# Windowed attention on one core: transposes two groups behind the scores, value products three groups behind

## The reference

```
scores = scale * np.matmul(q, k.transpose(0, 1, 3, 2))
keep = is_sink | in_window            # pos < n_sink, or 0 <= query - key < window
scores = np.where(keep, scores, -1000000000.0)
a = np.exp(scores - np.max(scores, axis=-1, keepdims=True))
a = a / (np.sum(a, axis=-1, keepdims=True) + 1e-09)
return np.matmul(a, v).astype(np.float32)
```

## Time and profile before

| | us |
|---|---|
| median of 3 runs | 871.35 (870.74 to 871.47) |
| the profiled execution, its own time | 870.85 |
| its span in the profile | 869.0 |
| TensorE busy in the span | 846.8 (97%) |
| VectorE busy | 615.8 (71%) |
| ScalarE busy | 400.8 (46%) |
| GpSimd busy | 170.0 (20%) |

### The profile page before, as it was taken

The page is one execution under the profiler, slowest core; times in us unless marked ns, Lnnn a source line. Parts: engine busy times, 40 slices in busy tenths (PEclk is TensorE's granted clock), DMA queues, the critical chain, the costliest instruction groups (busy, mean ns, idle before and its releaser), DMA issues.

```text
span 869.0 us, 13947 instructions
## 1 busy us (share of the span) xinstructions
PE 846.8 (97%) x4512; PEld 728.7 (84%) x4512; DVE 615.8 (71%) x1221; ACT 400.8 (46%) x739; POOL 170.0 (20%) x255
## 2 busy tenths in 40 slices
PE   5988999999999999999999999999999999999998
PEld 4666788888888888888999989998899989998896
DVE  6888779989898999885655656566565565655655
ACT  4888675445864457873144134224314314422410
POOL 4666410000110012231122022022012202202100
PEclk9999999999999999999999999999999999999999
DMA  7444550000780001861353154055135224313303
GB/s 252 142 141 131 141 143 4 2 1 16 169 196 7 0 0 38 173 128 30 86 117 57 58 115 88 27 115 115 23 91 115 48 66 115 74 41 66 67 1 148
DMA packets 25191, 72.72 MB, mean 84 GB/s; under 512 B 4288, under 2 KB 5952, under 8 KB 25152
## 3 DMA queue, kind: packets, MB, share of 16 engines
q0 software_dynamic: 10720, 33.82, 21.5%
q1 hardware_dynamic: 14288, 38.04, 13.0%
q10 hardware_dynamic: 144, 0.39, 0.2%
HBM read 35.28 MB, written 3.15 MB: 44 GB/s over the span
## 4 chain that ended last, share of the span: by engine, by line
PE 94%; ACT 2%; DVE 2%; issue 1%; DMA 1%; DVEq 0%; ACTq 0%
PE banks L877 30%; PE banks L803 27%; PE banks L774 15%; PE banks L598 15%; PE banks L613 2%; ACT pool L972 2%; PE banks L679 2%; PE banks L652 2%; PE banks L685 1%; DMA prm<-params 1%; DVE x_lo L1409 0%; DVE row_den L1399 0%; DVE pool L1389 0%; PE banks L655 0%; DVE mask L1300 0%
## 5 line engine op out<-in xcount | busy, mean ns | idle before, releaser
L1649 DVE SCALAR_TENSOR_TENSOR pool<-banks,p_norm,pool 128x512 f32<-128x512 f32 x180 | 133.5, 748 | 66.7 <-PE banks L877 64.9
L877 PE MATMUL banks<-w_hi,g_lo 128*128 128x512 f32 x384 | 150.6, 392 | 0.0
L877 PE MATMUL banks<-w_lo,g_hi 128*128 128x512 f32 x384 | 150.5, 392 | 0.0
L877 PE MATMUL banks<-w_hi,g_hi 128*128 128x512 f32 x384 | 149.3, 389 | 0.0
L1190 ACT ACTIVATE g_hi<-pool 128x384 fp32r<-128x384 f32 x96 | 50.5, 526 | 190.8 <-DVE pool L1629 139.2
L803 PE MATMUL banks<-x_hi,w_lo 128*128 128x384 f32 x256 | 86.0, 336 | 0.0
L803 PE MATMUL banks<-x_hi,w_hi 128*128 128x384 f32 x256 | 85.9, 335 | 0.0
L803 PE MATMUL banks<-x_lo,w_hi 128*128 128x384 f32 x256 | 85.8, 335 | 0.0
L877 PEld LDWEIGHTS banks<-w_hi,g_lo 128*128 128x128 f32 x384 | 72.0, 188 | 15.2
L877 PEld LDWEIGHTS banks<-w_hi,g_hi 128*128 128x128 f32 x384 | 72.2, 188 | 13.6
L877 PEld LDWEIGHTS banks<-w_lo,g_hi 128*128 128x128 f32 x384 | 72.0, 188 | 13.8
(11 more groups left out here) (136 smaller groups left out, 1743.0 us busy)
## 6 DMA issues: line engine op xcount, KB each, us to landing
w_raw<-weights SPq DMA_DIRECT2D x48, 512.0 KB, 4.4
w_lo<-w_raw POOLq DMA_DIRECT2D x48, 512.0 KB, 5.4
w_lo<-w_sum POOLq DMA_DIRECT2D x15, 384.0 KB, 4.0
pool<-kT SPq DMA_DIRECT2D x8, 400.0 KB, 4.2
pool<-v SPq DMA_DIRECT2D x8, 384.0 KB, 3.0
out<-pool SPq DMA_DIRECT2D x12, 256.0 KB, 2.4
pool<-qT SPq DMA_DIRECT2D x7, 384.0 KB, 3.4
w_lo<-pool POOLq DMA_DIRECT2D x2, 384.0 KB, 4.9
```

What stands on the lines that cost most here:

```text
L877: mm = pe.matmul(banks[:, bank, :], g[:, s, f * SUP + at:f * SUP + at + P], w_cols(w, p2 * SLOT + DOWN_AT[f], DM), start=(f == 0 and n == ...
L1649: dve.scalar_tensor_tensor(out=to, in0=d_bank, scalar=share, in1=to, op0=ALU.mult, op1=ALU.add)\
```

## The change

Transposes run two groups behind the scores instead of one (TURN_LAG = 2), value products three instead of two (VALUES_LAG = 3). A third probability buffer, prob_third, is laid into weight memory that is still unused then (w_hi from slot 6 on), so the exponentials of g wait for turn(g-3). GpSimd waits once for each group instead of once for each two units. VectorE's period has another order: copy_second(g-3) first, then masks 0 and 1 of g, the x_lo part for g-4 (at the end instead where it is the first part of a batch), one invert for all four units of g-1, masks 2 and 3. At the end, values(21) and turn(22) stand ahead of start_up(0), and ScalarE's copy_first(23) ahead of reciprocal(0).

```diff
+        prob_third = sb("prob_third", [P, 4 * WIDE + P], at=w_hi_at + mybir.dt.size(f32) * 6 * WC)
+        def group_prob(g):
+            return prob_third[:, :] if g % 3 == 2 else prob_w[:, g % 3, 0:4 * WIDE + P]
...
-                        if u % 2 == 0:
-                            pl.wait_ge(den_ready, ct * (UNITS // 2) + u // 2 + 1)
+                        if u % 4 == 0:
+                            pl.wait_ge(den_ready, ct * GROUPS_A + u // 4 + 1)
...
                     scores(ct, g)
-                    if at := group_at(ct, g, 2, before):
+                    if at := group_at(ct, g, VALUES_LAG, before):
                         values(*at)
-                    if at := group_at(ct, g, 1, before):
+                    if at := group_at(ct, g, TURN_LAG, before):
                         turn(*at)
...
+                values(CT - 1, GROUPS_A - 3)
+                turn(CT - 1, GROUPS_A - 2)
                 start_up(0)
...
-                            if u % 4 == 0 and ct * GROUPS_A + g >= 2:
-                                act.wait_ge(turned, 2 * (ct * GROUPS_A + g) - 2)
+                            if u % 4 == 0 and ct * GROUPS_A + g >= 3:
+                                act.wait_ge(turned, 2 * (ct * GROUPS_A + g) - 4)
...
-                        if at := group_at(ct, g, 1, ct > 0):
+                        if at := group_at(ct, g, TURN_LAG, ct > 0):
                             copy_first(*at)
-                        if at := group_at(ct, g, 2, ct > 0):
+                        if at := group_at(ct, g, VALUES_LAG, ct > 0):
                             take_after(*at)
...
+                copy_first(CT - 1, GROUPS_A - 2)
                 split_tile_hi(0, EARLY - 1, None)
                 split_tile_neg(EARLY - 1)
                 exponential(0)
                 take_after(CT - 1, GROUPS_A - 2)
+                copy_first(CT - 1, GROUPS_A - 1)
                 reciprocal(0)
-                copy_first(CT - 1, GROUPS_A - 1)
                 take_after(CT - 1, GROUPS_A - 1)
...
-                    for u in range(4 * g, 4 * g + 4):
-                        mask_scores(ct, u)
-                    invert(ct, 4 * g, 2)
-                    if at := group_at(ct, g, 3, before):
-                        take_after(*at)
-                    invert(ct, 4 * g + 2, 2)
+                    copied = group_at(ct, g, TURN_LAG + 1, before)
+                    ended = group_at(ct, g, VALUES_LAG + 1, before)
+                    first_half = ended is not None and ended[1] % (QT // 2) == 1
+                    if copied:
+                        copy_second(*copied)
+                    mask_scores(ct, 4 * g)
+                    mask_scores(ct, 4 * g + 1)
+                    if ended and not first_half:
+                        take_after(*ended)
                     if at := group_at(ct, g, 1, before):
-                        copy_second(*at)
+                        invert(at[0], 4 * at[1], 4)
+                    mask_scores(ct, 4 * g + 2)
+                    mask_scores(ct, 4 * g + 3)
+                    if first_half:
+                        take_after(*ended)
...
+                copy_second(CT - 1, GROUPS_A - 3)
+                invert(CT - 1, 4 * (GROUPS_A - 1), 4)
+                take_after(CT - 1, GROUPS_A - 4)
+                copy_second(CT - 1, GROUPS_A - 2)
                 start_gate(0)
```

More of the change, by code:

```diff
@@ L52 @@
 ADD_AT = [7 + 4 * n for n in range(EARLY - 1)]
+TURN_LAG, VALUES_LAG = 2, 3
 LAG = 3
@@ L133, in build @@
         x_lo = sb("x_lo", [P, CT, TOK], f32r)
+        w_hi_at = free_at[0]
         w_hi = sb("w_hi", [P, STEPS, WC], f32r)
@@ L186, in build @@
         rel = prob_w[:, 1, 4 * P:6 * P]
+        prob_third = sb("prob_third", [P, 4 * WIDE + P], at=w_hi_at + mybir.dt.size(f32) * 6 * WC)
+        def group_prob(g):
+            return prob_third[:, :] if g % 3 == 2 else prob_w[:, g % 3, 0:4 * WIDE + P]
         def window_prob(u, w):
             at = WIDE * (u % 4) + (P if u % 4 >= 2 else 0)
-            return prob_w[:, u // 4 % 2, at:at + w]
+            return group_prob(u // 4)[:, at:at + w]
         prob_T = part(TURNED_AT, 4, 512)
@@ L457, in window_attention @@
                             pl.wait_ge(prob_ready, ct * UNITS + u + 1)
-                            sinks = prob_w[:, group % 2, P:P + 4 * WIDE].rearrange("p (a b) -> p a b", a=4)[:, :, 0:SINKS]
+                            sinks = group_prob(group)[:, P:P + 4 * WIDE].rearrange("p (a b) -> p a b", a=4)[:, :, 0:SINKS]
                             pl.tensor_copy(sink_prob[:, group % 2, :, :], sinks).then_inc(sinks_ready, 1)
```

## The result

The changed kernel takes 861.61 us (861.33 to 861.70, 4 runs) against 871.05 us (870.28 to 871.47, 4 runs): ratio 0.9892, 95% interval 0.9875 to 0.9909, so 9.4 us less. 11.5 were forecast; the time lies in the range, and on the side on which the gain is smaller. The profiled execution took 861.70 us, its span 859.9.

A forecast was written before the change was run, and what follows sets the result against it. TensorE, busy 97%, bounds the kernel; only its attention waits can go. Ramp 24.35 + six batches at 10.1 + end 2.5 = 87.45 us to start_up(0), against 98.93: 11.5 less, so 859.8 us, range 857 to 865.5.

The forecast's parts named there:

- TensorE's floor of 9.95 a batch: Attention's steady part: TensorE's steps without any wait sum to 9.95 us a batch, where 11.70 was measured before.
- the ping-pong on VectorE: Steady part before: VectorE stands in invert for exponentials of the same g, while ScalarE waits 14.7 us for masks.
- ScalarE's copy: copy_first out of the type 0 (narrow) period: done at 3.9, wanted at 3.96, margin nothing; charged 0.15 us a batch.
- the x_lo wait: TensorE's waits at L652 for the x_lo part, 6.5 us in seven; forecast to go, with 1.0 us margin.
- VectorE's work: Six inverts a batch become three, saving 1.0 us: busy 10.05 becomes 9.05 a batch, under TensorE's 9.95.
- The walk: Step-by-step timing of VectorE and ScalarE through one period of the new order, from its start on TensorE.
- ScalarE's copy late: Rival, chance 0.10: the type 0 margin becomes a third of a microsecond lost each period, 11.0 a batch, 865.2 us.
- The ramp: Periods 0 to 3, bound by ScalarE's and VectorE's chain: period 6 would start at 24.35 us instead of 28.70.
- The end: values(21), turn(22) and a 0.5 us wait for turn(21)'s copies between period 23 and start_up(0): together 2.5 us.
- Queues and weights at nothing: SyncE's later k load and the weight tiles, wanted 11.5 us earlier but issued 9.3 earlier, were costed at nothing.
- The port rival: Chance 0.08: every invert collides with a GpSimd multiply on the shared port, VectorE 10.5 a batch, 862.8 us.
- The x_lo wait stays, or slower: Two rivals: TensorE's x_lo wait remains, 869.5 us, chance 0.06; a two-period ring makes TensorE await copy_first, 874.9, chance 0.04.

## Why the prediction was right, point by point

- **TensorE's floor of 9.95 a batch**: right; 9.94 in the kernel with the earlier copy.
- **What holds before, the ping-pong on VectorE**: right, and shown by two kernels: with the inverse of the own group a batch stays at 11.27 to 11.30 even at the new lags. Of the 1.75 us that a batch lost before (11.70 against 9.95), the lags alone removed 0.4 (11.30), the new order with them 0.96 more (10.34), and the last 0.4 hung on the place of ScalarE's copy (9.94). The prediction named the x_lo wait and the ping-pong side by side. That the first is where the second comes out at TensorE fits the lags alone, where it was still 4.0 us, but is argued.
- **VectorE's work**: 9.05 busy us a batch were forecast, 51.76 / 6 = 8.63 came. The term that was mis-sized is the saved inverses: L1399 was charged at its median, 0.169, but its mean before was 0.250, since 15 of the 48 took over 0.2 us. "Once 0.661" is a misreading of the earlier trace rows, which gives the longest and not how many were long. "It doesn't bind" holds for its total, not for its order: 0.33 us more in front of mask 2 cost 0.38 a batch.
- **ScalarE's copy**: the place was right (a margin of nothing out of the narrow period), the size was not: charged with 0.15 us a batch, it cost 10.34 - 9.94 = 0.40, still inside the stated bounds (9.95 to 10.5 a batch). The walk has the exponentials done at about 3.4 after the narrow period's start and the copy at 3.9. In the timeline above the period starts at 25.39 and the copy, 29.21 + 0.57, ends at 4.4: mask 2 starts at 27.75, 0.35 us behind the walk. The walk gave each of the two narrow masks 0.21 us, from start to next start they take 0.40 and 0.31, so the x_lo part begins 0.32 late (why they take longer is not shown); and 0.16 us of issue lie ahead of mask 2. This is the rival "ScalarE's copy late" at somewhat over a third of its size (0.40 of 1.05 a batch).
- **The ramp**: 25.39, not 24.35. The step that failed is "as the masks now run ahead of them". The masks could not run ahead: the scores have four banks, each row of scores waits for the mask four rows back, and a row that TensorE starts out of idleness comes late. TensorE begins the first wide row at 9.31 and the mask of that row starts at 10.80; in the steady part all four rows of a group take 1.11.

```profile
10.80 0.44 DVE L1399 CUSTOM_DVE_ANT_0 pool<-banks,mask 128x272 f32<-128x272 f32 x1 [0.51 <-ACT pool L981]
...
14.62 0.52 ACT L981 ACTIVATE prob_third<-pool,row_min 128x272 f32<-128x272 f32 x1
...
15.32 0.52 ACT L981 ACTIVATE prob_third<-pool,row_min 128x272 f32<-128x272 f32 x1
15.85 0.36 ACT L992 ACTIVATE pool<-banks 128x256 f32<-128x256 f32 x1
```

  Group 2's exponentials end at 15.85 instead of 15.0, and the first copy comes late with them; period 4 starts at 18.29, where the walk has 17.25. The profile names ScalarE for the first of these waits, but its exponential was through by 9.7; that the scores were the ones awaited is read from the program's order and from when TensorE made them, not tested.
- **The end**: 2.55 against 2.5. Right. Moving start_up ahead, in the kernel with the earlier copy, won nothing.
- **Queues and weights at nothing**: right; TensorE has no idle time from 89.98 to 115.00, and the stretch from just behind the first start_up product to the end of the span is 769.9 us long (90.0 on), 770.0 before (99.0 on).
- **The port rival**: it did not come as priced. L1409, the former L1399, ran 24 times at 157/166/487 ns (shortest, median, longest):

```profile
L1409 DVE TENSOR_SCALAR row_den<-row_sum x24: 157/166/487, 11.5 to 88.1; 128x4 f32<-128x4 f32 x24
```

  Five were long, 0.36 to 0.49 us, two of them in the steady part; with a mean of 0.19 us there the excess is 0.02 x 18 = 0.4 us of VectorE's time. Before, the same excess was (0.250 - 0.169) x 37 = 3.0 us, so the change made collisions fewer. They are not what makes the ring long: in the kernel with the inverse of the own group one of 24 is over 0.2 us (0.23), and a batch still takes 11.27. What they cost at the old lags was not measured.

  The Trainium skill's rule on the shared ports (SBUF — State Buffer, Who interferes with whom) has the later of a two-port VectorE instruction and a GpSimd instruction wait for the whole of the earlier one. This trace agrees in part: all five long ones start inside a multiply of GpSimd, but four others, which start in the last 0.15 us of one (at 29.96, 50.73, 61.05 and 71.37), took 0.17.
- **The x_lo wait stays, or slower**: neither came. The lags alone are near the first (870.0 us against 869.5), though with a shorter wait and by VectorE's ring. Of the second no kernel was made: two buffers are slower by a ring of one period, not by that of two periods which the prediction named.

In sum, the mechanism was as forecast. The two misses, 1.04 in the ramp and 1.44 in the batches, lie on the same side, so nothing cancelled; they made the gain 9.4 us instead of 11.5.

## What to carry to other kernels

Here the deeper pipeline paid only once no engine stood still inside a period for a result of that same period. Look for the ring that closes within one engine's round (here mask, exponential, inverse, mask) before adding a stage, and for what a stage needs (here a third buffer) before counting on it. When an engine's totals fit but with little slack, the order inside its round decides: one instruction moved by one place was worth a third of what the whole change brought. In the ramp, cost an engine that starts out of idleness by rows from such a place, not by its steady pace.

## What the runs showed of the hardware

TensorE's granted clock fell where it idled much in attention. In the kernel with the order alone (columns as in the earlier trace rows):

```profile
80.00:84.00 4.00, 1.71 (x13) 1.13 (x13) 1.36 (x8) 3.29 (x10) 2.67 (x5) 0.97 0.57 201
84.00:88.00 4.00, 4.00 (x35) 3.18 (x36) 2.40 (x12) 2.05 (x9) 2.20 (x4) 0.61 0.00 0
```

TensorE had worked 1.71 of the 4 us before, and then got 0.61 of full speed over 4 us, so most of that time at the lower level, 1.2 GHz. The narrow group's scores in it take 1.66 us, where they take 0.93 at the upper level:

```profile
83.78 1.66 PE L620 MATMUL banks<-pool 64*128 64x128 f32 x8
```

So in this kernel the stalls were paid for twice. Little work alone does not decide it: from 48 to 50 us the same kernel worked 0.52 of 2 us, and the clock stayed at 1.00 behind it. In the steady part of the changed kernel, with waits of at most 0.5 us, the clock stays at 1.00. With two buffers, where TensorE was idle as much (busy 13.2 to 14.0 of each 20 us from 20 to 100), it stayed at 1.00 there too, and fell only at the end of attention (0.97 from 100 to 122 us). What made the difference between these two stays open.
